# Splitting the phi projection of a linear attention into three fp32r products

## What is computed

```python
# q, k, v: (batch 4, heads 8, seq 576, head_dim 64); w_phi: (64, 128); all float32
def phi(x):
    proj = np.einsum('bhsd,df->bhsf', x, w_phi)
    proj = proj - np.max(np.abs(proj), axis=-1, keepdims=True)
    return np.concatenate([np.exp(proj), np.exp(-proj)], axis=-1)
q_p, k_p = (phi(q), phi(k))
kv = np.einsum('bhsf,bhsd->bhfd', k_p, v)
z = np.sum(k_p, axis=2)
num = np.einsum('bhsf,bhfd->bhsd', q_p, kv)
den = np.einsum('bhsf,bhf->bhs', q_p, z)[..., None] + 1e-06
return (num / den).astype(np.float32)
```

## Time and profile before

| | |
|---|---|
| runs | 1034.8, 1035.58, 1033.31 us |
| the profiled execution | 1034.8 us, its span 1032.9 us |
| mean granted TensorE clock | 0.982 |
| TensorE products | 987.6 us busy, 96% of the span |
| VectorE, ScalarE, GpSimd | 40%, 27%, 15% |

### The profile page before, as it was taken

The page is one execution under the profiler, slowest core; times in us unless marked ns, Lnnn a source line. Parts: engine busy times, 40 slices in busy tenths (PEclk is TensorE's granted clock), DMA queues, the critical chain, the costliest instruction groups (busy, mean ns, idle before and its releaser), DMA issues.

```text
span 1032.9 us, 19572 instructions
## 1 busy us (share of the span) xinstructions
PE 987.6 (96%) x6575; PEld 885.6 (86%) x6576; DVE 410.3 (40%) x966; ACT 278.8 (27%) x558; POOL 159.2 (15%) x219
## 2 busy tenths in 40 slices
PE   9999999999999999999999999999866999999995
PEld 6898989999989898989899998989654888888884
DVE  4555576674314131313222231423554322443621
ACT  3444333333222122212122222212413122332410
POOL 6773000003300000000000000000002222232331
PEclk9999999999999999999999999999978999999998
DMA  8677022312110100000000001000551111513310
GB/s 223 183 199 208 11 78 82 86 61 93 47 42 1 41 0 20 20 10 30 10 30 10 30 0 41 0 21 1 184 184 31 41 45 46 195 43 126 112 33 20
DMA packets 54207, 68.16 MB, mean 66 GB/s; under 512 B 28319, under 2 KB 36639, under 8 KB 54177
## 3 DMA queue, kind: packets, MB, share of 16 engines
q1 hardware_dynamic: 47616, 45.21, 14.4%
q0 software_dynamic: 6560, 22.56, 7.1%
HBM read 54.11 MB, written 14.69 MB: 67 GB/s over the span
## 4 chain that ended last, share of the span: by engine, by line
PE 93%; DMA 2%; DVE 2%; issue 1%; ACT 0%; SPq 0%; POOL 0%; POOLq 0%; DVEq 0%; ACTq 0%
PE bank L1050 30%; PE bank L1071 14%; PE bank L1193 10%; PE bank L1174 10%; PE bank L956 7%; PE bank L969 7%; PE bank L1009 6%; PE bank L999 2%; PE bank L1186 2%; PE bank L1087 1%; DMA scale_rows<-r_scale 1%; PE bank L1080 1%; PE bank L1157 1%; DMA e_w<-w 1%; PE bank L1040 1%
## 5 line engine op out<-in xcount | busy, mean ns | idle before, releaser
L744 DVE TENSOR_TENSOR prod<-silu,bank 128x256 f32<-128x256 f32 x108 | 45.5, 421 | 247.5 <-ACT silu L520 247.5
L1050 PE MATMUL bank<-x_hi,wg_hi 128*128 128x256 f32 x432 | 125.2, 290 | 0.2 <-issue 0.2
L1050 PE MATMUL bank<-x_hi,wv_hi 128*128 128x256 f32 x432 | 122.3, 283 | 0.0
L1050 PE MATMUL bank<-x_lo,wv_hi 128*128 128x256 f32 x432 | 122.3, 283 | 0.0
L1050 PE MATMUL bank<-x_hi,wv_lo 128*128 128x256 f32 x432 | 122.2, 283 | 0.0
L1050 PE MATMUL bank<-x_hi,wg_lo 128*128 128x256 f32 x432 | 122.2, 283 | 0.0
L1050 PE MATMUL bank<-x_lo,wg_hi 128*128 128x256 f32 x432 | 122.1, 283 | 0.0
L520 ACT ACTIVATE silu<-bank 128x256 f32<-128x256 f32 x108 | 41.4, 383 | 252.7 <-PE bank L1050 252.7
L1071 PE MATMUL bank<-wo_hi,h_hi 128*128 128x512 f32 x216 | 85.9, 397 | 0.0
L1071 PE MATMUL bank<-wo_hi,h_lo 128*128 128x512 f32 x216 | 84.3, 390 | 0.0
L1071 PE MATMUL bank<-wo_lo,h_hi 128*128 128x512 f32 x216 | 84.2, 390 | 0.0
(11 more groups left out here) (185 smaller groups left out, 1843.4 us busy)
## 6 DMA issues: line engine op xcount, KB each, us to landing
e_w<-w SPq DMA_DIRECT2D x32, 512.0 KB
stage<-w_out POOLq DMA_DIRECT2D x16, 384.0 KB, 3.7
k_sb<-kT SPq DMA_DIRECT2D x8, 576.0 KB, 4.8
x_in<-x_rows SPq DMA_DIRECT2D x9, 512.0 KB, 3.6
y_rows<-y_sb SPq DMA_DIRECT2D x18, 256.0 KB, 2.0
v_sb<-v SPq DMA_DIRECT2D x32, 128.0 KB, 5.3
q_sb<-qT SPq DMA_DIRECT2D x16, 256.0 KB, 2.9
x_rows<-x_sb SPq DMA_DIRECT2D x16, 256.0 KB, 2.1
```

What stands on the lines that cost most here:

```text
L744: dve.tensor_tensor(prod[:, c % 2, :], silu[:, c % 2, :], bank[2 + c % 2][:, 0:GT], ALU.mult).then_inc(prod_ready, 1)
L1050: mm = pe.matmul(acc[:, 0:GT], w[:, k, cols], x[:, k, :], start=(k == 0 and i == 0), stop=(k == KC - 1 and i == 2))
```

## The change

The projection's operands are split as the MoE's are.

- `phi` gets a high part (ScalarE, once) and a low part (VectorE, once); `phi_split` tells TensorE.
- Each tile of keys or queries gets a high part `in_hi` on ScalarE (`input_high`, called for step n+2 ahead of the exponentials of step n) and a low part `in_lo` on VectorE (`input_low`, called for step n+1 between the reduce and the difference of step n). The helper `later` names the step that follows, over the batches' and the stages' ends. Both tiles have two halves.
- `project` makes three fp32r products for each pair of heads, and waits for `in_lo_ready`. The waits on `k_in` and `q_in`, the landing of the inputs, go from TensorE to ScalarE.

```diff
-        phi = sb("phi", [P, 2, F], F32, a_ctx)
+        phi_hi = sb("phi_hi", [P, 2 * F], F32R, a_ctx)
+        with ExitStack() as phi_ctx:
+            phi = sb("phi", [P, 2, F], F32, phi_ctx)
+        phi_lo = sb("phi_lo", [P, 2 * F], F32R, a_ctx)
+        in_hi, in_lo = (sb(n, [P, 2, 2, P], F32R, a_ctx) for n in ("in_hi", "in_lo"))
...
+        def later(src, b, n, last):
+            if n >= STEPS:
+                n -= STEPS
+                if not last:
+                    b = b + 1
+                elif src is k_sb:
+                    src, b = q_sb, 0
+                else:
+                    return None
+            order = (steps() if src is k_sb else qsteps())[n]
+            return src, b, b * STEPS + ((0 if src is k_sb else KSTEPS) + n), *order
...
         def _(act):
+            def input_high(step):
+                if step is None:
+                    return
+                src, b, N, n, q, j = step
+                r, s = ROWS[j], n % 2
+                if src is k_sb and j == 0:
+                    act.wait_ge(k_in[q], b * 16 + 16)
+                if src is q_sb and q == 0:
+                    act.wait_ge(q_in[j], b * 16 + 16)
+                act.activation(in_hi[:, s, :, 0:r], src[:, 2 * q:2 * q + 2, j * P:j * P + r], ACT.Copy
+                               ).then_inc(in_hi_ready, 1)
+
+            act.wait_ge(phi_in, 32)
+            act.activation(phi_hi[:], phi[:].rearrange("p a f -> p (a f)"), ACT.Copy).then_inc(phi_split, 1)
+            input_high(later(k_sb, 0, 0, False))
+            input_high(later(k_sb, 0, 1, False))
...
                     act.wait_ge(dif_ready, b * STEPS + (n + 3))
+                    input_high(later(k_sb, b, n + 2, last))
                     act.wait_ge(mm_done, b * STEPS + (n + 1))
...
                     act.wait_ge(proj_done, b * STEPS + (KSTEPS + n + 1))
+                    input_high(later(q_sb, b, n + 2, last))
                     act.wait_ge(qt_done, b * STEPS + (n + 1))
...
         def _(dve):
-            def differences(N, n, r):
+            def input_low(step):
+                if step is None:
+                    return
+                src, b, N, n, q, j = step
+                r, s = ROWS[j], n % 2
+                dve.wait_ge(in_hi_ready, N + 1)
+                dve.tensor_tensor(in_lo[:, s, :, 0:r], src[:, 2 * q:2 * q + 2, j * P:j * P + r], in_hi[:, s, :, 0:r],
+                                  ALU.subtract).then_inc(in_lo_ready, 1)
+
+            def differences(N, n, r, following):
...
                 dve.tensor_reduce(amax[0:r, s], proj, AX.X, ALU.max, apply_absolute_value=True
                                   ).then_inc(amax_done, 1)
+                input_low(following)
                 dve.wait_ge(amax_done, N + 1)
...
+            dve.wait_ge(phi_split, 1)
+            dve.tensor_tensor(phi_lo[:], phi[:].rearrange("p a f -> p (a f)"), phi_hi[:], ALU.subtract
+                              ).then_inc(phi_split, 1)
+            input_low(later(k_sb, 0, 0, False))
             k_batch(0, True)
...
-            def project(src, b, N, n, q, j):
+            def project(N, n, j):
                 r, s = ROWS[j], n % 2
-                if src is k_sb and j == 0:
-                    pe.wait_ge(k_in[q], alone(pe, b * 16 + 16))
-                if src is q_sb and q == 0:
-                    pe.wait_ge(q_in[j], alone(pe, b * 16 + 16))
+                pe.wait_ge(in_lo_ready, alone(pe, N + 1))
                 pe.wait_ge(dif_ready, alone(pe, N + 1))
                 for pair in range(2):
-                    mm = pe.matmul(bank[s][0:r, pair * 2 * F:(pair + 1) * 2 * F], src[:, 2 * q + pair, j * P:j * P + r],
-                                   phi[:].rearrange("p a f -> p (a f)"), start=True, stop=True)
+                    for i, (x, w) in enumerate(((in_hi, phi_hi), (in_hi, phi_lo), (in_lo, phi_hi))):
+                        mm = pe.matmul(bank[s][0:r, pair * 2 * F:(pair + 1) * 2 * F], x[:, s, pair, 0:r], w[:],
+                                       start=(i == 0), stop=(i == 2))
                 mm.then_inc(proj_done, 1)
```

More of the change, by code:

```diff
@@ L183, in build @@
         q_in = [sem(f"q_in{j}") for j in range(JS)]
+        phi_split = sem("phi_split")
+        in_hi_ready = sem("in_hi_ready")
+        in_lo_ready = sem("in_lo_ready")
         proj_done = sem("proj_done")
@@ L609, in k_batch @@
                     dve.wait_ge(exp_done, b * STEPS + (n + 1))
-                    differences(b * STEPS + n, n, ROWS[j])
+                    differences(b * STEPS + n, n, ROWS[j], later(k_sb, b, n + 1, last))
                     if n == 3 and not first:
@@ L658, in q_batch @@
                         dve.wait_ge(exp_done, KSTEPS + n + 1)
-                    differences(b * STEPS + (KSTEPS + n), n, ROWS[j])
+                    differences(b * STEPS + (KSTEPS + n), n, ROWS[j], later(q_sb, b, n + 1, last))
                     if first and n == 1:
@@ L977, in k_batch @@
                 for n, q, j in every:
-                    project(k_sb, b, b * STEPS + n, n, q, j)
+                    project(b * STEPS + n, n, j)
                     if first and n < 4:
@@ L987, in _ @@
             keep_warm(7, 12)
-            pe.wait_ge(phi_in, 32)
+            pe.wait_ge(phi_split, 2)
             k_batch(0, True)
@@ L1015, in q_batch @@
                 for n, q, j in every:
-                    project(q_sb, b, b * STEPS + (KSTEPS + n), n, q, j)
+                    project(b * STEPS + (KSTEPS + n), n, j)
                     if first and n < 2:
```

## The result

The changed kernel takes 1105.2 us (median of 4 runs, 1091.1 to 1109.1), the kernel before 1034.9 (1033.3 to 1035.6): a ratio of 1.060 with a 95% interval of 1.050 to 1.069. Forecast were 1036.0 us, with 1041.5 as the upper end. The prediction was wrong by 69 us. Three more executions took 1088.6, 1101.2 and 1114.9 us.

A forecast was written before the change was run, and what follows sets the result against it. TensorE was taken to bound both attention stages. Blocked key steps and start +7.2, free key steps -2.2, casts +0.6, query steps -4.8, short tiles +0.3 gave +1.1 us: 1036.0 us, range 1030 to 1041.5.

The forecast's parts named there:

- the clock rival: Key stage: TensorE's clock falls to 1.2 GHz in steps blocked by GpSimd, 5.1 us each, up to 21 us; chance 0.02.
- the locked steps: Key steps whose low part waits behind GpSimd's subtraction: 3.58 us each, TensorE idle for 1.05 us of it.
- TensorE's gain: Projection: six fp32r products take 0.80 us instead of 0.92, saving 0.12 us a step, 9.6 us over 80 steps.
- The lock with GpSimd: Key stage: VectorE's low part waits out GpSimd's subtraction on the shared port, making steps 3.58 us; 7.1 us lost.
- the 14 steps: Key steps from the ninth to the 23rd, beside GpSimd's splitting: 45.9 us instead of 38.8, 7.1 us more.
- Casts block: Key stage: GpSimd's casts also block low parts, by the skill page; eight casts without subtraction add 0.6 us (bounds 0 and 4.8).
- Loads moved to another engine's wait: ScalarE waits for keys and queries one step earlier than TensorE did; loads land in time, so no cost.
- Hidden low part: Attention: the low part delays nothing, leaving the gains, -8.6 us, 1026.2 us; chance 0.25, whole or half.
- the lock that never lets go: Key stage: weight loads always in time, all 16 pieces hold a step, +6.4 us, 1041.2 us; chance 0.30, casts included.
- fp32r doesn't cost more than it seems: Projection: the rival had unhidden weight loads making each fp32r product cost 0.20 us, giving +22 us; chance 0.03.
- a clock below 1.00 before 240 us: Attention: granted clock under full speed, listed as a sign that the forecast is wrong.
- a MoE stage that begins much more than 1 us later: Start of the MoE stage shifted much more than 1 us, later or earlier; listed as a sign of a wrong forecast.

The follow-up runs named there:

- p2: Changed kernel, GpSimd's splits held back until the keys are done, plus one made TensorE pause behind the seventh projection; 1112.7 us.
- b1: Kernel before the change, with only GpSimd's splits of the MoE weights held back until the keys are done; 1035.7 us, ratio 0.9993.
- e9: Changed kernel with low parts two steps ahead, keys loaded earlier, and the query stage's low part behind the copy of the last sums; 1020.2 us, ratio 0.9857.
- e4: Changed kernel with one extra 128x512 product on ones in each later key step; 1036.7 us, ratio 1.0017.
- e2: Changed kernel with all splits and waits, but the projection's old fp32 products on unsplit tiles; 1060.2 us (1048.6 and 1071.7).
- e1: Changed kernel with the low part made two steps ahead, behind the difference, ScalarE's high part moved with it; 1026.9 us, ratio 0.9913 from three of five runs.
- e7: Changed kernel with the low part two steps ahead and key loads issued once high and low parts have read them; 1027.5 us, ratio 0.9913.
- e3: Changed kernel with GpSimd's splits of the MoE weights held back until the keys are done; 1029.2 us, ratio 0.994.
- e6: Changed kernel with the low part two steps ahead and GpSimd's splits held back until the keys are done; 1031.4 us, ratio 0.996.
- e8: Changed kernel with low parts two steps ahead, earlier key loads and one extra product on ones per key step; 1033.8 us, ratio 0.9995.
- p1: Changed kernel with the old fp32 products, GpSimd's splits held back, and one made TensorE pause behind the seventh projection; 1080.4 us.
- p3: Changed kernel, GpSimd's splits held back, one made TensorE pause behind the seventh projection, one extra product on ones per key step; 1050.2 us.

## Why the prediction was wrong

**The step that failed is the clock rival**: "over 14 steps up to 21 us", with a chance of 0.02. It was what happened. Mis-sized was not the step under a low clock (5.1 us forecast, 4.75 measured) but how many there are: I tied the low clock to the locked steps, so that it would end with the pauses. The runs show it isn't tied to them. At half clock TensorE has no pause left at all, and yet the clock stayed down for 34 steps; p2 shows the same behind one single pause. The sum by the rival's own form would have been 34 x (4.75 - 2.77) = +67 us. And its small chance rested on "no row of the attention shows it". The attention before has a single pause of that length behind its first projections, the 1.10 us ahead of 11.70, at 1.00; b1 shows that the same pause can also bring the clock down. One pause was little evidence about 14 in a row, and the range should have been wider.

**TensorE's gain: right, and a little small.** Six products take 0.79 us (0.80 forecast); undisturbed steps take 2.49 us with keys (2.53) and 2.94 with queries (2.97). That is 0.16 and 0.15 us a full step where 0.12 was forecast, and 0.20 us on average over the last 36 query steps. e9, 15 us below before, shows the gain in the time, and more of it than the 9.6 us forecast; where the rest of a step's gain comes from wasn't looked into.

**The lock with GpSimd: right as a mechanism, too large as a sum.** Blocked low parts end 0.28 to 0.29 us behind GpSimd (forecast 0.29), a locked step takes 3.58 us (3.58). But the 14 steps lost less than the 7.1 us forecast: in e4 42.5 us against 39.0, so 3.5 with the added products and 0.4 if all of their time is taken off; in e2, with fp32 products and so without the gain of 14 x 0.12, 2.8 (41.8 against 39.0). The lock let go after some three steps of each half batch. Casts block as well (42.92 above), which no row of before had shown. The Trainium skill ("SBUF — State Buffer", section "SBUF: two separate sides") speaks of a lock held for the whole instruction, for a VectorE instruction with two SBUF inputs against whatever GpSimd instruction reads SBUF; the rows agree for both.

**Loads moved to another engine's wait, "I cost this at nothing": wrong.** In e1 this wait paused TensorE 1.23 us, and the clock fell 1.4 us behind it; in the profile of the changed kernel, at the slower pace, no such pause stands.

**The rivals.** Hidden low part (1026.2 us) is what e7 and e1 built (1027.5 and 1026.9); the lock that never lets go wasn't seen in a key stage; fp32r doesn't cost more than it seems at full clock. Of the signs named, "a clock below 1.00 before 240 us" and "a MoE stage that begins much more than 1 us later" came, and both were listed as proving the forecast wrong.

**Left open.** What made the clock fall at 28.85 us, the fall that cost the 69 us. In the 13 us ahead of it TensorE had idled only twice, 0.21 and 0.19 us; the longer pauses (1.31 and 1.02 us) ended at 9.34 and 11.76, where it fell for the first time. Pauses of 1.0 to 2.1 us went either way. At the start, e3 had 1.57, 1.03 and 1.03 us at 1.00, e9 1.57, e7 2.07; b1 fell behind 1.10 and e2 behind 2.13. Each pause of 2.27 us and more behind the start had a fall beside it (e6, e7, e8, p1 to p3). Holding the splits back took the fall away (e3, two executions), but e9 keeps them beside the key stage and doesn't fall, so they don't do it by themselves. That it goes by TensorE's pauses is inferred from the falls right behind one, and the fall at 28.85 doesn't fit it well. How short a pause suffices with which products wasn't tried. Executions of the changed kernel differ by 26 us (1088.6 to 1114.9) as their time at half clock does (132 to 203 us by the estimate); why that differs is open.

## What to carry to other kernels

When a change replaces long products by shorter ones on an engine that is fully busy, look for every pause it opens on TensorE and price a pause by the time the clock may take to come back, not by its own length. Here it paid more to make inputs two steps ahead than to guard with extra products. Follow each wait that moves to another engine to the load behind it. A chain in which untouched TensorE lines grow, with TensorE 100% busy, is a clock and not a wait: read the granted clock first.

## What the hardware showed that I had not expected

- TensorE at 1.2 GHz for 167 us while its records are 100% busy, with fp32r products 128x256 and fp32 products 128x65 in turn. Behind one pause of 4.1 to 4.4 us it was 174 us with these, 65 us with fp32 products in place of fp32r, 17 us with one 128x512 product on ones more per step (one execution each). Among fp32r key steps without products on ones it didn't come back in any profile; among query steps it did.
- The same mix held 2.4 GHz for 93 us without a pause (e3), and for 99 us with one of 1.6 us at their start (e9): with one and the same work both levels last.
- One 128x512 product on ones per key step (0.22 us) was worth some 69 us in the changed kernel and cost 6 us in one whose key stage had no pause behind its start (e7, e8).
